# Expert output transposed on chip into the MLP input, rows placed by an indirect DMA at the end, MLP weights split on GpSimd

## What is computed

```python
q_pool = q.reshape(B, H, S // 2, 2, D).mean(axis=3)
attn = softmax(scale * q_pool @ k.T)          # per batch and head
x = (attn @ v).transpose(0, 2, 1, 3).reshape(1152, 512)

e_idx = argmax(x @ w_gate, axis=1)            # one expert per token
for e in range(8):
    ye = maximum(x[mask] @ w1[e], 0) @ w2[e]
    out[mask] = gate_w * sigmoid(x @ w_output_gate)[mask, e] * ye

h = out @ w_in
g = h * tanh(log1p(exp(minimum(h, 20))))      # h itself above 20
return g @ w_out
```

## Time and profile before

| | us |
|---|---|
| median of 3 runs (718.06 to 721.94) | 719.09 |
| the profiled execution | 722.0 |
| its span, first to last instruction | 720.4 |
| PE busy | 677.3 (94%) |
| DVE busy | 506.9 (70%) |
| ACT busy | 405.9 (56%) |
| POOL busy | 89.9 (12%) |
| mean granted clock of PE | 0.984 |

### The profile page before, as it was taken

One profiled execution on the slowest core, in us unless ns is written; L12 is line 12 of the kernel. 1 busy time (PEld: TensorE's weight loads), 2 busy tenths in 40 slices (PEclk: granted clock), 3 DMA queues, 4 the chain that ended last, 5 costly groups with the idle time before them and its releaser, 6 DMA issues.

```text
span 720.4 us, 14720 instructions
## 1 busy us (share of the span) xinstructions
PE 677.3 (94%) x5141; PEld 598.0 (83%) x5142; DVE 506.9 (70%) x1155; ACT 405.9 (56%) x808; POOL 89.9 (12%) x123
## 2 busy tenths in 40 slices
PE   4899999999999999979999999993799999999997
PEld 3788888888888888778998999982698999899895
DVE  4667676777677775746655656666799978777874
ACT  4566566656666667335654655555566645455543
POOL 2313140404041200310000000005000000000000
PEclk9999999999999999989999999996999999999999
DMA  8378989797967500389952993104100010001001
GB/s 223 89 188 239 269 217 254 174 253 170 264 151 203 133 3 1 111 299 400 398 225 57 333 358 112 44 29 116 45 1 1 0 45 2 1 0 45 1 0 45
DMA packets 92385, 99.00 MB, mean 137 GB/s; under 512 B 41584, under 2 KB 65136, under 8 KB 91824
## 3 DMA queue, kind: packets, MB, share of 16 engines
q1 hardware_dynamic: 87984, 86.81, 40.9%
q0 software_dynamic: 2480, 8.13, 3.2%
q10 hardware_dynamic: 1872, 3.41, 1.5%
HBM read 62.16 MB, written 19.66 MB: 114 GB/s over the span
## 4 chain that ended last, share of the span: by engine, by line
PE 88%; DVE 4%; ACT 2%; another core or an unknown queue 2%; DMA 1%; issue 1%; POOL 0%; SPq 0%; ACTq 0%; POOLq 0%; DVEq 0%
PE score_banks L1020 13%; PE score_banks L983 13%; PE turn L772 12%; PE pvT L753 11%; PE score_banks L997 10%; PE score_banks L729 5%; PE score_banks L730 5%; PE score_banks L1037 4%; PE turn L1037 4%; PE pvT L1037 4%; PE turn L701 1%; PE turn L970 1%; PE turn L779 1%; PE score_banks L736 1%
## 5 line engine op out<-in xcount | busy, mean ns | idle before, releaser
L772 PE MATMUL turn<-ident,prob 128*128 128x128 f32 x648 | 111.6, 282 | 3.4 <-DVE probT L1320 2.5
L1256 DVE TENSOR_REDUCE nmax_part<-score_banks 128x1 f32<-128x768 f32 x72 | 69.0, 958 | 60.8 <-PE score_banks L730 47.4
L983 PEld LDWEIGHTS score_banks<-xsT,w_slot 128*128 128x128 f32 x832 | 97.2, 197 | 7.8 <-issue 7.0
L983 PE MATMUL score_banks<-xsT,w_slot 128*128 x832 | 98.3, 280 | 5.7 <-ACT xsT L1154 4.1
L772 PEld LDWEIGHTS turn<-ident,prob 128*128 128x128 f32 x648 | 77.6, 142 | 25.3 <-issue 13.6
L1066 ACT ACTIVATE prob<-score_banks,nmax 128x1152 f32<-128x1152 f32 x72 | 87.6, 1217 | 3.8 <-DVE nmax L1266 3.7
L753 PE MATMUL pvT<-probT,v_sb 128*64 128x128 f32 (+1 forms) x1404 | 85.9, 269 | 0.0
L1463 DVE TENSOR_TENSOR w_lo<-w_slot,w_hi 128x512 fp32r<-128x512 f32 x104 | 71.8, 693 | 19.3 <-ACT w_hi L1169 19.2
L1073 ACT ACTIVATE probT<-turn 128x384 f32<-128x384 f32 x72 | 35.4, 492 | 88.5 <-PE turn L772 88.4
L729 PE MATMUL score_banks<-kT,qT 128*128 128x384 f32 x192 | 81.4, 424 | 4.1 <-DVE qT L1285 3.5
L753 PEld LDWEIGHTS pvT<-probT,v_sb 128*64 128x64 f32 x1404 | 69.5, 137 | 11.8 <-issue 11.8
(11 more groups left out here) (216 smaller groups left out, 1352.0 us busy)
## 6 DMA issues: line engine op xcount, KB each, us to landing
w_slot<-moe_w SPq DMA_DIRECT2D x16, 2048.0 KB, 13.7
slots_dram<-zeros SPq DMA_DIRECT2D x8, 1408.0 KB, 10.8
raw_k<-k SPq DMA_DIRECT2D x16, 288.0 KB, 6.0
v_sb<-v SPq DMA_DIRECT2D x16, 288.0 KB, 4.3
raw_q<-q SPq DMA_DIRECT2D x16, 256.0 KB, 3.9
w_in_sb<-moe_w_in SPq DMA_DIRECT2D x1, 4096.0 KB, 13.3
w_out_sb<-moe_w_out SPq DMA_DIRECT2D x1, 4096.0 KB, 14.5
kT<-k_hi SPq DMA_DIRECT2D x14, 288.0 KB, 4.5
```

The source lines that it names most:

```text
L772: last = pe.transpose(bank[:, j * P:(j + 1) * P], prob[:, s % 2, c * KC + j * P:c * KC + (j + 1) * P], ident[:, :])
L983: last = pe.matmul(h1_bank[f % 4][:, 0:P], w1_e[:, d, f * P:(f + 1) * P], xsT[:, d, bass.ds((t % XS_RING) * P, P)], start=(d == 0), stop=( ...
L1256: dve.tensor_reduce(nmax_part[:, s, 0:1], scores[s % 2][:, lo:lo + 2, 0:KC], AX.XY, ALU.max, negate=True).then_inc(max_part, 1)
```

## The change

- DVE also computes `tile_cols`: the column of each expert tile in an x2T that is sorted by expert and holds no gaps. x2T_hi and x2T_lo get room for N + 128 columns. A tile always writes 128 columns; what it writes past its expert's tokens is overwritten by the next tile.
- In each tile PE transposes the y of the tile before out of `y_sb` (`turn_y`) into PSUM, between `fill_xs` and the second matmuls. ACT and DVE write `x2T_hi` and `x2T_lo` from there (`x2_high`, `x2_low`), ahead of w2 pieces 4 to 7. The store to DRAM and the gathers go. The last tile is turned after the first `hidden`.
- POOL scatters, by nine indirect DMAs of 4 bytes a token, the output row of each token to its sorted place in `order_dram`; SP loads the list into `out_idx`. Output tiles leave by indirect DMAs on POOL.
- w_in and w_out are loaded in halves of 2 MB into ring slots 0 to 3, when experts 4, 5, 6 and 7 are done. POOL splits them (cast, then subtraction), w_in in 4 pieces of 2048 columns, w_out in 16 pieces of 512.
- The ring of xsT goes from 4 to 2 tiles, and several buffers move.

```diff
@@ SP, after the expert loads
-            wait_expert(RING)
-            sp.dma_start(w_in_sb[:, :, :], w_in.rearrange("(t p) f -> p t f", p=P)).then_inc(w_in_landed, 16)
-            wait_expert(RING + 1)
-            sp.dma_start(w_out_sb[:, :, :], w_out.rearrange("(t p) d -> p t d", p=P)).then_inc(w_out_landed, 16)
+            for n in range(2):
+                wait_expert(RING + n)
+                sp.dma_start(w_in_sb[n][:, :, :], w_in_rows[:, n * HALF:(n + 1) * HALF, :]).then_inc(w_in_landed[n], 16)
+            for n in range(2):
+                wait_expert(RING + 2 + n)
+                sp.dma_start(w_out_sb[n][:, :, :], w_out_rows[:, n * HALF2:(n + 1) * HALF2, :]).then_inc(w_out_landed[n], 16)
@@ POOL
-            with pool.Fori(0, tiles) as t:
...
-                pool.dma_start(slots_dram[bass.ds(row, P), :], y_sb[:, :]).then_inc(y_stored, 16)
...
-                pool.indirect_dma_start(x_tok[:, i, :], None, slots_dram,
-                                        bass.IndirectOffsetOnAxis(slot_idx[:, i:i + 1], 0)).then_inc(y_back[i], 16)
+            pool.wait_ge(sorted_ready, 1)
+            for i in range(TPH):
+                pool.indirect_dma_start(order_dram, bass.IndirectOffsetOnAxis(sorted_idx[:, i:i + 1], 0),
+                                        out_row[:, i:i + 1], None).then_inc(order_stored, 16)
+
+            for d in range(DT):
+                n, m = d // HALF, d % HALF
+                pool.wait_ge(w_in_landed[n], 16)
+                pool.tensor_copy(w_in_hi[n][:, m, :], w_in_sb[n][:, m, :]).then_inc(win_hi_ready, 1)
+                pool.wait_ge(win_hi_ready, d + 1)
+                pool.tensor_tensor(w_in_lo[n][:, m, :], w_in_sb[n][:, m, :], w_in_hi[n][:, m, :].bitcast(F32), ALU.subtract
+                                   ).then_inc(win_lo_ready, 1)
+            for f in range(FT2):
...
+                pool.tensor_copy(w_out_hi[n][:, m, :], w_out_sb[n][:, m, :]).then_inc(wout_hi_ready, 1)
+                pool.wait_ge(wout_hi_ready, f + 1)
+                pool.tensor_tensor(w_out_lo[n][:, m, :], w_out_sb[n][:, m, :], w_out_hi[n][:, m, :].bitcast(F32), ALU.subtract
+                                   ).then_inc(wout_lo_ready, 1)
...
+                pool.indirect_dma_start(out, bass.IndirectOffsetOnAxis(out_idx[:, i:i + 1], 0),
+                                        y_out[:, i % TC, :], None).then_inc(out_landed, 16)
@@ PE
+            def turn_y(t):
+
+                pe.wait_ge(y1_copied, t + 1)
+                pe.wait_ge(x2_lo_ready, t + 1)
+                for d in range(DT):
+                    last = pe.transpose(x2_bank[:, d * P:(d + 1) * P], y_sb[:, d * P:(d + 1) * P], ident[:, :])
+                last.then_inc(x2_filled, 1)
...
-                fill_xs(t + FILL_AHEAD, fill_bank[0], stage[:, FILL_AHEAD, :])
-                pe.wait_ge(y1_copied, t + 1)
+                fill_xs(t + FILL_AHEAD, fill_bank[0], stage)
+                turn_y(t)
...
-            for i in range(TC):
-                fill_x2(i)
-            pe.wait_ge(x2_lo_ready, TC)
+            pe.wait_ge(x2_lo_ready, tiles + 1)
             pe.wait_ge(win_lo_ready, DT)
-            for f in range(AHEAD):
+            hidden(0, 0)
+            turn_y(tiles)
+            for f in range(1, AHEAD):
                 hidden(0, f)
-                for i in later_fills[f]:
-                    fill_x2(i)
@@ ACT, in each tile
                 copy_xs(t + FILL_AHEAD, fill_bank[0], (t + FILL_AHEAD) % XS_RING)
+                x2_high(t)
                 for f in range(W2_RING, FT1):
                     w2_high(f)
@@ DVE, in each tile
                 look_ahead(n)
+                x2_low(t)
                 for f in range(W2_RING, FT1):
                     w2_low(f)
```

More of the change, by code:

```diff
@@ L276, in build @@
         xs_stored = sem("xs_stored")
-        stage_landed = [sem(f"stage_landed{n}") for n in range(FILL_AHEAD + 1)]
+        stage_landed = sem("stage_landed")
         xs_filled = sem("xs_filled")
@@ L1000, in _ @@
             expert_tiles(pe, pe_expert)
-            def fill_x2(i):
-                pe.wait_ge(y_back[i], 16)
-                if i >= 3:
-                    pe.wait_ge(x2_lo_ready, i - 2)
-                bank = x2_fill_bank[i % 3]
-                for d in range(DT):
-                    last = pe.transpose(bank[:, d * P:(d + 1) * P], x_tok[:, i, d * P:(d + 1) * P], ident[:, :])
-                last.then_inc(x2_filled, 1)
+            tiles = pe.value_load(bounds[0:1, NE:NE + 1], min_val=NE, max_val=SLOT_TILES)
             def hidden(c, f):
@@ L1187, in _ @@
             tiles = act.value_load(bounds[0:1, NE:NE + 1], min_val=NE, max_val=SLOT_TILES)
[L1188 to L1197 removed]
+            act.wait_ge(stage_landed, 16 * tiles + 16)
             def h2_exponential(c, f):
@@ L1226, in mlp_chunk @@
                     rough_recip(c, f)
-                    if first:
-                        for i in later_fills[f]:
-                            x2_high(i)
                     if f + 1 < FT2:
@@ L1233, in mlp_chunk @@
                         h2_exponential(c + 1, 0)
-                    if first:
-                        act.activation(w_out_hi[:, f, :], w_out_sb[:, f, :], ACT.Copy).then_inc(wout_hi_ready, 1)
                     if f:
@@ L1239, in mlp_chunk @@
                         g_high(c - 1, FT2 - 1, False)
-            for i in range(TC):
-                x2_high(i)
-            act.wait_ge(w_out_landed, 16)
             h2_exponential(0, 0)
+            x2_high(tiles)
             for c in range(CHUNKS):
@@ L1452, in _ @@
-            then(dve.tensor_reduce(ended[:, :, 0], row_of[:, :, :], AX.X, ALU.add))
-            dve.tensor_copy(tile_rows[:, :], ended[:, :, 0]).then_inc(rows_ready, 1)
-            dve.sem_inc(y1_copied, 1)
-            dve.sem_inc(y_sb_free, 1)
-            dve.sem_inc(h1_ready, 4)
+            then(dve.tensor_tensor(begins_at[:, :, :, :], begun[:, :, :].unsqueeze(2).broadcast_to([P, ROW_TILES, 2, NE]),
+                                   starts_of[:, :, :].unsqueeze(1).broadcast_to([P, ROW_TILES, 2, NE]), ALU.mult))
@@ new lines, in _ @@
+            then(dve.tensor_reduce(tile_at_f[:, :, :], begins_at[:, :, :, :], AX.X, ALU.add))
+            then(dve.tensor_tensor(tile_pos[:, :, :], tile_at_f[:, :, :], tile_step[:, :, :], ALU.add))
+            dve.tensor_copy(tile_rows[:, :], tile_pos[:, :, 0])
+            dve.memset(tile_cols[:, 0:1], 0)
+            dve.tensor_copy(tile_cols[:, 1:], tile_pos[:, :, 1]).then_inc(rows_ready, 1)
+            then(dve.tensor_tensor(to_sorted[:, :], sorted_start[:, 0:NE], row_start[:, :], ALU.subtract))
@@ new lines, in _, with x2_low @@
+            dve.memset(y_sb[:, :], 0.0).then_inc(y1_copied, 1)
+            dve.sem_inc(x2_lo_ready, 1)
+            dve.sem_inc(h1_ready, 4)
+            def x2_low(t):
+                col = dve.value_load(tile_cols[0:1, bass.ds(t, 1)], min_val=0, max_val=N)
+                dve.wait_ge(x2_hi_ready, t + 1)
+                dve.tensor_tensor(x2T_lo[:, :, bass.ds(col, P)], x2_bank[:, :].rearrange("p (d n) -> p d n", d=DT),
+                                  x2T_hi[:, :, bass.ds(col, P)].bitcast(F32), ALU.subtract).then_inc(x2_lo_ready, 1)
@@ L1536, in mlp_chunk @@
                     mish_numer(c, f)
+                    if first and not f:
+                        x2_low(tiles)
                     if f >= 2:
@@ L1547, in mlp_chunk @@
                         mish_gated(*before)
-                    if first:
-                        for i in later_fills[f]:
-                            x2_low(i)
-                    if first:
-                        dve.wait_ge(wout_hi_ready, f + 1)
-                        dve.tensor_tensor(w_out_lo[:, f, :], w_out_sb[:, f, :], w_out_hi[:, f, :].bitcast(F32),
-                                          ALU.subtract).then_inc(wout_lo_ready, 1)
                     if f == COPY_STEP and not first:
```

227 lines of the change are left out of this document (123 added, 104 removed).

## The result

The changed kernel takes 753.25 us (median of 4 runs, 752.45 to 754.83) against 719.25 in the same set: 1.0475 times the kernel before, 95% interval 1.0448 to 1.0501. The forecast was 743.5, slower, with a range of 706 to 762. The profiled execution took 753.26, its span 751.3, so 30.8 us more than before.

A forecast was written before the change was run, and what follows sets the result against it. PE was taken to bound the kernel everywhere but at the joint. Span 720.4 - 23.6 + 5.2 + 0.5 + 20 + 5 + 10 + 5 + 2.3 = 744.8, + 1.6 around it, less 2.9: 743.5 us, range 706 to 762.

The forecast's parts named there:

- The joint: From the last expert matmul's end to the MLP's first output matmul: 12.1 us instead of 35.7, -23.6.
- turn_y: Four more transposes in each of 13 expert tiles, between `fill_xs` and the second matmuls: 0.4 us each, +5.2.
- The weight split: POOL's split makes DVE operations reading two SBUF operands stand until POOL's instruction ends: w_in +20, w_out +5 and +10.
- the clock: PE idle over 4 us at each w_in half drops to its lower clock: twice 2.5, +5 (0 to 8).
- the first half of w_out: Short holds of `w2_low` in expert 7's first tile and some of the next: +5 (2 to 8).
- The phase argument: POOL starts on w_in's first half as the next tile reaches its second phase; `w2_low(4)` is due 2.2 us later.
- The MLP: Second half of w_out: DVE held behind POOL, steps about 9 us instead of 4.2 for 2.7 steps, +10 (5 to 14).
- Routing, the list: Before the first expert tile, extra DVE operations: +0.5 (0 to 2); output-order scatters and index load fit idle queue time: nothing.
- The tail: End of kernel: POOL issues three indirect output DMAs, the last from about 718.9, landing 4.1 us later: +2.3 (0 to 5).
- B: Rival: only part of the holds' cost appears, as phases miss or POOL is held: 15 to 30 us, 719 to 731; chance 0.17.
- C: Rival: worse holds, or low clock through a whole tile: another 15 to 25 us, 760 to 770; chance 0.08.
- Rival A: DVE's holds beside POOL's weight split don't cost: 40 us go, 703.5 us, -2.2%; chance 0.18.

## Why the prediction was right, and where it was not

*The joint* (-23.6, measured -23.5): right in its parts: 1.1 us idle, which holds the copy of y, then five hiddens and a `turn_y`.

*turn_y* (+5.2, measured +7.8): a plain tile is 0.60 longer, not 0.40. The first phase, which now ends with eight transposes instead of four, grew by 0.45 (366.75 to 374.73, against 341.32 to 348.85 before: 7.98 and 7.53), the second by about 0.15. Costing the chain to w2 piece 4 at 0 was nearly right.

*The weight split.* Its mechanism was right, and nearly every sign put forward for it came: maxima of up to 5.0 us in the two tiles that were named, 24.9 us each where some 23 were forecast, and the holds got short with short POOL instructions and were gone when POOL only wrote or did nothing there. One sign was off: a held `w2_low` doesn't end with POOL's instruction but 0.55 us behind it. +25 with the clock was forecast for w_in, 22.9 measured (what part of it is the clock's wasn't separated); +5 for the first half of w_out, 3.2 measured. The phase argument held: POOL starts on the first half 2.2 us before piece 4 is due, as forecast, and on the second 3.2 us before.

*The MLP* (+10, measured +5.9): the mis-sized term is the length of a step. I took 9 us, with a whole POOL instruction behind each of six DVE operations. One step, from `numer` to `numer`, lasts 7.13 (DVE and POOL; other engines' lines are left out):

```profile
547.71 1.52 DVE L1537 SCALAR_TENSOR_TENSOR numer<-expo 128x384 f32<-128x384 f32 x1
548.76 0.94 POOL L709 CAST w_out_hi<-w_out_sb 128x512 fp32r<-128x512 f32 x1
549.16 0.96 DVE L1542 TENSOR_TENSOR g_lo<-prod,g_hi 128x384 fp32r<-128x384 f32 x1
549.78 1.48 POOL L711 TENSOR_TENSOR w_out_lo<-w_out_sb,w_out_hi 128x512 fp32r<-128x512 f32 x1
550.04 1.64 DVE L1554 SCALAR_TENSOR_TENSOR resid<-numer,rough 128x384 f32<-128x384 f32 x1
...
552.48 0.54 DVE L1549 SCALAR_TENSOR_TENSOR prod<-score_banks,numer 128x384 f32<-128x384 f32 x1
552.95 1.17 DVE L1563 SCALAR_TENSOR_TENSOR prod<-resid,ratio 128x384 f32<-128x384 f32 x1
...
554.84 1.51 DVE L1537 SCALAR_TENSOR_TENSOR numer<-expo 128x384 f32<-128x384 f32 x1
```

The alternation is exact, six POOL instructions to a step, and the operation fed from PSUM (552.48) is free of it. But part of each operation lies beside the other engine's. 16/6 = 2.7 steps, each 2.9 longer than 4.2, are 7.8; 5.9 were measured, so some 2 of it found slack, where I had taken off 3.

*Routing, the list* (+0.5 and 0, measured -0.3 and +10.6): here the forecast had a term at nothing without a reason that covers it: the sentence that the scatters and the index load "fall where both queues have time". The queues of POOL and SP had time; what I hadn't asked is what 1152 elements of 4 bytes do to the transfers beside them. Moving them took 11.8 us off the first two tiles. The start of the first tile lies between 309.9 and 314.4 in the executions of this case, so neither -0.3 nor +0.5 can be read as an effect.

*The tail* (+2.3, measured +4.0): the three issues came as forecast, the last 3.4 us after the last matmul. It landed in 2.7 us, sooner than the gather's 4.1 that I had used; but I had left out POOL's DRAIN of 2.27 us behind it, and so the end is 5.4 us after that issue. My own numbers, 718.9 + 4.1 against 720.4, would have given +2.6.

*The sum* was 6.4 us short in the span: the list's 10.6, tiles 2.6 and tail 1.7 on one side; 2.1 for w_in with its clock, 1.8 for w_out, 4.1 for the MLP and 0.8 for the start on the other (rounding and what lies between the parts make up the rest). That the total came as near as it did is in part luck: the overlooked list was more than half paid for by 8.8 us that I had charged too much elsewhere. The rest of the 9.75 us to the median is that I took 2.9 us off for a profiled run above its median, while the changed kernel's stood at its median, and that 2.0 us lie around its span, not 1.6.

Some bounds were added up wrongly. The bounds of the parts give a plain sum of 720 to 766, not 731 to 758; B's 15 to 30 us give 718.5 to 733.5, C's 15 to 25 give 758.5 to 768.5. The measured time is outside A and B and inside the parts' range either way. Rival A, that the holds don't cost, has fallen: short instructions, writing alone and taking the split away each took most or all of the holds away, and the time with them.

## What to carry to other kernels

An idle GpSimd is no free engine for elementwise work while VectorE has two-operand work in SBUF on or near the critical path: look for VectorE's small SBUF operations that grow beside GpSimd's, and price each meeting at the rest of the other's instruction. If it must be GpSimd, use short instructions: here a quarter of the length took 16 us off. And when a small table goes through DRAM by elements, ask which transfers of tiles are on their way at that moment. If the last DMAs of a kernel move to another engine's queue, look at what that engine still has to do behind their landing.

## What the runs showed of the hardware

- The hold works both ways, and where both engines have work waiting they alternate: POOL's 2048-column cast took 1.90 us unheld and 2.35 behind a held `w2_low`, its 512-column subtraction 1.29 and 1.61.
- POOL writing 2048 columns without reading (an iota, 1.85 us) did not hold a two-operand DVE operation at all: 0.694 us at most.
- Nine scatters of 128 elements of 4 bytes to DRAM took 14.1 us each (median) to land beside 2 MB loads, and a 256 KB load among them 10.6 instead of 2.9; the 4.5 KB read back took 15.7 us there and 3.8 alone.
- With the last DMAs on GpSimd's queue, a DRAIN of 2.27 us (2.28 with plain DMAs) stood between their landing and the end of the span; with them on SP's queue POOL's DRAIN was over at 510.1, beside other work, and the span ended 0.4 us after the last landing.
- PE's granted clock fell to 0.50 within 4.08 us of idleness in the midst of a tile, and stayed there through two short bursts of matmuls and the start of a third, to about 450.
